# Identity matmuls beside the routing's vector steps, and the first cast of x moved ahead of a register reading

## What is computed

```python
# attention: B, H, S, D = 4, 8, 576, 64; its output x is [4, 576, 512]
logits = np.einsum('bsd,de->bse', x, w_gate)              # 8 experts
local_gate = 1.0 / (1.0 + np.exp(-np.einsum('bsd,de->bse', x, w_local).squeeze(-1)))
for b in range(B):
    prev_e = -1
    for s in range(S):
        fresh_e = int(np.argmax(logits[b, s]))
        if s == 0 or local_gate[b, s] < 0.5:
            e = fresh_e
        else:
            e = prev_e if prev_e >= 0 else fresh_e
        prev_e = e
        # p = softmax(logits[b, s])
        h = np.maximum(x[b, s] @ w1[e], 0.0)              # 512 -> 1024
        out[b, s] = p[e] * (h @ w2[e])                    # 1024 -> 512
```

## Time and profile before

| what | value |
|---|---|
| median of three runs | 727.08 us |
| profiled execution | 727.54 us |
| its span, first to last instruction | 725.7 us |
| mean granted TensorE clock | 0.967 of full speed |
| TensorE matmul / VectorE / ScalarE / GpSimd busy | 91% / 52% / 47% / 27% of the span |

### The profile page before, as it was taken

One profiled execution on the slowest core, in us unless ns is written; L12 is line 12 of the kernel. 1 busy time (PEld: TensorE's weight loads), 2 busy tenths in 40 slices (PEclk: granted clock), 3 DMA queues, 4 the chain that ended last, 5 costly groups with the idle time before them and its releaser, 6 DMA issues. The chain is left out here.

```text
span 725.7 us, 13847 instructions
## 1 busy us (share of the span) xinstructions
PE 657.4 (91%) x4323; PEld 525.1 (72%) x4323; DVE 377.1 (52%) x781; ACT 341.0 (47%) x705; POOL 196.4 (27%) x172
## 2 busy tenths in 40 slices
PE   4776799999999999999955799999999999999994
PEld 1222678888888888888735688888888888888883
DVE  4998465555555555555757632269523432222220
ACT  4896656666666666666530342267424422222221
POOL 3000344444444444445511011113211121111101
PEclk9998999999999999999985699999999999999998
DMA  3997814447544444444074824146411111111100
GB/s 81 209 226 168 180 33 99 99 99 203 111 98 99 99 99 98 98 99 98 16 252 159 304 86 146 43 159 252 146 43 43 36 44 43 43 43 43 43 0 1
DMA packets 68183, 77.04 MB, mean 106 GB/s; under 512 B 46767, under 2 KB 47279, under 8 KB 68144
## 3 DMA queue, kind: packets, MB, share of 16 engines
q1 hardware_dynamic: 63392, 64.58, 34.2%
q0 software_dynamic: 4080, 11.54, 4.9%
q10 hardware_dynamic: 672, 0.44, 0.2%
HBM read 69.06 MB, written 11.27 MB: 111 GB/s over the span
## 5 line engine op out<-in xcount | busy, mean ns | idle before, releaser
L791 DVE CUSTOM_DVE_ANT_0 sm<-ps_s,bias 128x576 f32<-128x576 f32 x128 | 91.7, 754 | 68.8 <-PE ps_s L1063 68.8
L611 ACT ACTIVATE sm<-sm,negmax 128x576 f32<-128x576 f32 x144 | 111.9, 778 | 7.0 <-DVE negmax L791 6.9
L1238 PE MATMUL ps_pv<-w2hi,hThi 128*128 128x512 f32 x200 | 80.5, 402 | 1.3 <-DVEq L980 1.3
L1000 DVE TENSOR_TENSOR hTlo<-ps_s,hThi 128x512 fp32r<-128x512 f32 x50 | 32.2, 686 | 95.1 <-ACT hThi L725 95.1
L1238 PE MATMUL ps_pv<-w2hi,hTlo 128*128 128x512 f32 x200 | 78.3, 392 | 0.0
L1238 PE MATMUL ps_pv<-w2lo,hThi 128*128 128x512 f32 x200 | 78.0, 390 | 0.0
L1134 PE MATMUL ps_pv<-pT,vt 128*64 128x320 f32 (+1 forms) x512 | 69.2, 410 | 4.3 <-DVE pT L814 0.6
L506 POOL CAST ksplit<-raw 128x1152 fp32r<-128x1152 f32 x15 | 17.2, 1146 | 204.8 <-DMA raw<-in_kq_dram 204.8
L1216 PE MATMUL ps_s<-w1hi,xThi 128*128 128x512 f32 x200 | 66.1, 412 | 7.2 <-DVE w1lo L967 3.7
L558 POOL DMA_INDIRECT out_dram<-ysb,sidx x25 | 26.7, 1070 | 153.0 <-ACT ysb L732 153.0
L717 ACT ACTIVATE hsb<-ps_s 128x512 f32<-128x512 f32 x25 | 14.9, 598 | 113.1 <-PE ps_s L1216 113.1
(11 more groups left out here) (180 smaller groups left out, 1279.0 us busy)
## 6 DMA issues: line engine op xcount, KB each, us to landing
w1raw<-in_moe_w_dram SPq DMA_DIRECT2D x18, 1024.0 KB
w2raw<-in_moe_w_dram SPq DMA_DIRECT2D x18, 1024.0 KB
raw<-in_kq_dram SPq DMA_DIRECT2D x32, 432.0 KB, 5.3
bias<-stage SPq DMA_DIRECT2D x32, 288.0 KB, 4.6
raw<-in_kq_dram SPq DMA_DIRECT2D x32, 128.0 KB, 5.1
vt<-in_v_dram SPq DMA_DIRECT2D x32, 128.0 KB, 2.5
tokens_dram<-xl SPq DMA_DIRECT2D x64, 64.0 KB, 1.7
bias_tail<-stage SPq DMA_DIRECT2D x4, 144.0 KB, 2.4
```

Source lines behind the costliest of these rows:

```text
L611: nc.scalar.activation(probs, probs, ACT.Exp, scale=-1.0, bias=negmax[:, u % 2, hd:hd + 1], accum_out=sums[:, pr % 2, 2 * t + hd:2 * t + h ...
L791: nc.vector.tensor_tensor_reduce(sm[:, u % 2, S * hd:S * (hd + 1)].rearrange("p (a c) -> p a c", a=2), ps_s[:, hd, :, 0:HALF], bias.rearra ...
L1000: V.tensor_tensor(hTlo[:, 4 * i:4 * i + 4, :].rearrange("p k t -> p (k t)"), ps_s[:, 1, i, :], hThi[:, 4 * i:4 * i + 4, :].bitcast(F32).re ...
L1238: last = nc.tensor.matmul(ps_pv[:], h[:, f, :], w[:, f, :], start=f == 0 and h is hThi and w is w2hi, stop=f == KF - 1 and h is hTlo)
```

## The change

TensorE gets a helper `beside(first, last, n)`: for each step count from `first` to `last - 1` it waits until `route` has it and then multiplies `ident` by itself, 128x128 in f32, into `ps_pv`, which nothing reads there; at the last count it does so `n` times. It is called ahead of the turn of `hold` (one matmul), ahead of the turn of `code` (three), behind that turn (three and five), and behind the counts (twelve and three). After the 20 probability matmuls of L1193 and ahead of `turn_x(0, 0, 0)` stand twelve more, without waits. The scan that makes `prefix` gets the name `counts`. On ScalarE `xt_hi(0)` and on VectorE `xt_lo(0)` move ahead of the wait for `tiles_told` and the register reading.

```diff
@@ scalar
             split_hi(-1, None, w2_in_e, w2hi, w2raw, w2_hi, None)
+            xt_hi(0)
             act.wait_ge(tiles_told, 1)
...
             split_changed(changed, 0, run, w1_in, w1hi, w1raw, w1_hi, h_done)
-            xt_hi(0)
@@ vector
-                                      0.0, ALU.mult, ALU.add))
+                                      0.0, ALU.mult, ALU.add), "counts")
...
+            xt_lo(0)
             dve.wait_ge(tiles_told, 1)
...
             split_changed(changed, 0, slot, w1hi, w1lo, w1raw, w1_lo, w1_hi, h_done)
-            xt_lo(0)
@@ tensor
+            def beside(first, last, n=1):
+
+                for count in range(first, last):
+                    pe.wait_ge(route, count)
+                    for _ in range(n if count == last - 1 else 1):
+                        nc.tensor.matmul(ps_pv[:, 0:P], ident[:], ident[:], start=True, stop=True)
             pe.wait_ge(tables, 12)
             for n, name, dst, turned in ((1, "hold", ps_t, hold_turned), (0, "code", ps_s[:, 0], codes_turned)):
+                beside(1 if n else AT["hold"] + 2, AT[name])
                 pe.wait_ge(route, AT[name])
...
+            beside(AT["code"] + 3, AT["chosen"], 5)
             pe.wait_ge(route, AT["chosen"])
...
                              start=True, stop=True).then_inc(counted, 1)
+            beside(AT["counts"], AT["places0"], 3)
             for c in range(BT):
...
             last.then_inc(probs_placed, 1)
+
+            for _ in range(12):
+                nc.tensor.matmul(ps_pv[:, 0:P], ident[:], ident[:], start=True, stop=True)
```

## The result

The changed kernel takes **730.21 us**, the median of 17 runs (727.25 to 732.45), against 727.08 for the kernel before on the same occasions (17 runs, 724.95 to 728.94). The ratio is 1.004, with a 95% interval of 1.0025 to 1.0056: slower by 0.4%, where 0.5% (730.7 us) was forecast. The profiled execution took 731.4 us around a span of 729.6; before it was 727.54 around 725.7.

What follows compares the result with a forecast made beforehand. TensorE's first hidden matmul was taken to set the end: 398.96 + 4.3 (twelve fills) - 0.5 (turn) - 0.2 (casts) = 402.6, +3.6 us on 727.08, so 730.7 us; 8-in-10 range 723.6 to 732.0.

Steps and rivals of the forecast that it cites:

- The bound: Expert stage: TensorE's first hidden matmul, at 398.96, sets the end; whatever moves it moves the end as much.
- The price of a fill: Each 128x128 f32 filling matmul on TensorE: 0.22 us at the high clock, 0.43 us at the low.
- Part 1: Fills around the turns of hold and code: the clock falls, slow fills delay the turn of chosen, onehot 1.1 us later.
- Part 2: Fifteen fills behind the counts: no charge, gidx's 0.56 us wait on TensorE disappears; gidx +0.5 us in sum, at 390.3.
- Part 3: Twelve fills ahead of the turn of x: probability matmuls stay at the low clock, the turn starts 4.3 us later.
- Part 4: The turn of x itself: at the high clock behind the fills, 0.6 us in place of 1.11, -0.5 us.
- Part 5: Casts ahead of register readings: VectorE's reading stays in the way, 3.3 us from turn's end against 3.48, -0.2 us.
- Part 6: Clock in tiles 0 and 1: lost in the idle gaps, they pay 2.9 and 2.8 us again; change 0.
- Rival A: Routing: the clock never falls, probability matmuls at half the price; -3.1 us together, 724.0 us; chance 0.29.
- Rival B: Fills' delay paid, but the clock outlives the idle 3.3 us and tile 0 takes 5.5 us; 727.8 us; chance 0.16.

Runs made afterwards that it cites:

- a1: The changed kernel without the twelve fills ahead of the turn of x; 726.87 us, ratio 1.000 to the kernel before.
- a4: The kernel before with only the `beside` fills around the first turns and behind the counts, casts unmoved; 728.33 us, ratio 1.0013.
- c1: The changed kernel with all its fills, but both casts of x moved back behind the register readings; 726.94 us, ratio 1.0007 to the kernel before.
- a3: The kernel before with only the casts of x moved ahead of the register readings; 726.59 us, ratio 0.9998.
- a2: The kernel before with only the twelve fills ahead of the turn of x; 726.12 us, ratio 0.9994.
- d4: The changed kernel with eight more fills behind the turn of x; 728.70 us, ratio 1.0021 to the kernel before.
- d1: The kernel before with only eight fills behind the turn of tile 0's x and fourteen behind tile 0's transposes; 722.71 us, ratio 0.9944.
- b2: The kernel before with only fourteen fills behind tile 0's transposes, ahead of tile 1; 724.89 us, ratio 0.9983.
- b1: The changed kernel without its twelve fills, with eight behind the turn of x and fourteen behind tile 0's transposes; 722.95 us, ratio 0.9956 to the kernel before.

## Why the prediction was right, point by point

- **The bound** (398.96 moves the end). Right: the start of tile 0 moved by 3.62 us, the span by 3.9. Of the 3.62 us, 0.32 came from attention, which the sum (+3.6) did not have; from the routing's first matmul it is 3.3.
- **The price of a fill**, 0.22 and 0.43 us. Right: eight fills took 2.03 us at the high clock from 375.05 to 377.08 (0.25 each, as they wait for steps between), and the twelve 4.98 us, 0.42 each.
- **Part 1**, the clock lost at 373.9 and onehot 1.1 us late. Wrong for the profiled execution, where the clock held and onehot came 0.3 us earlier behind the logits; the judgement that failed there is "I judge no". Right for the other six traces of kernels with these fills, where the clock had fallen by 374.1 (a1 and a4: onehot 1.0 and 1.2 us later). The profiled execution is the exception.
- **Part 2**, gidx at 390.3. It came at 389.38: the 0.56 us of waiting is gone, as said, and Part 1's delay did not come. In c1, where it came, gidx was 0.4 us later behind the logits than in the kernel before (said: 0.5).
- **Part 3**, the decisive one: probability matmuls at the low price in spite of the fills before them (0.214 us each), and the turn at 398.7. It came at 398.67, and the exact agreement is luck: two errors of 0.7 us cancel. The fills began 0.7 us earlier and took 5.0 us instead of 4.3, for the clock came back about 4.7 us into them (398.4) and not after 3.5. The 3.5 was a reading of the row from 70 to 73; the dense work there begins at 69.38 in the trace, so the clock came back after 4.1 us.
- **Part 4**, 0.6 us for the turn. Right.
- **Part 5**, 3.3 us from the turn's end, VectorE's reading in the way. Right (the row's 3.31 us of idle time), and a3 shows the worth of the move as 0.17 us (said: 0.2).
- **Part 6**, tile 0 and tile 1 as before. Right in size (8.56, 8.35) for the profiled execution. But the prediction booked this as no change, where a2, c1 and d4 show that much of the loss lies here: the twelve fills would have given the clock to tile 0 if the moved cast had not made the idle stretch behind the turn long enough to lose it. Of the loss of 0.4% (2.9 us), c1 takes away 2.4 us and d4 1.4. The sum had +4.3 for the fills and -0.2 for the cast; behind the late turn the moved cast is no gain but costs 1.7 us of start (3.91 us from the turn's start against 2.23 in c1) and the clock. Neither part alone shows a cost (0.9994 and 0.9998).
- **Rival A** needed the clock high through the probability matmuls. It was high from 385 and fell at 388.1, in the placing matmuls ahead of them. **Rival B** did not happen in the profiled execution. It happened in a2 and c1, and the five short runs of the changed kernel (727.25 to 727.76 us, clock 0.985) are at its time (727.8), so it probably happened in these too; without a trace that is not shown. The median of 730.21 is then that of a mixture in which the forecast's course had the larger share, and its closeness to 730.7 is in part luck.

## What to carry to other kernels

A fill ahead of awaited work is free only where the engine would wait longer than the fills take at the clock that they will have. Eight fit into 3.48 us even at the low clock (d1: 3.47 us); fourteen fit into 3.71 us only because the clock was high in them (3.29 us in b2; at 0.43 us each it would be 6.0). Put them behind the last work that someone waits for, not ahead of it. Filling has to reach to the start of the dense work that is to profit: an idle stretch between the fills and that work can take back what they bought. And when a step is moved ahead of another on one engine, look for what the other one releases: here a semaphore behind a register reading.

## What the runs showed of the hardware

- Executions of one program differ by several us, and the mean granted clock goes with it. Of the changed kernel's 17 runs the five shortest (727.25 to 727.76 us) have 0.985, the two longest (732.45 and 732.33 us) 0.970 and 0.972. The kernels whose two gaps are filled spread over 0.6 (d1), 1.2 (d2) and 2.1 us (b1), in six runs each.
- A few full-size matmuls between steps did keep the clock at 1.00 for eight us in one execution (373 to 381, TensorE's rows busy for 6.13 of 8.00 us), and in none of the six other traces with the same or nearly the same fills. Why was not tried.
- The 20 matmuls of 52 columns (the probabilities), one behind the other, ran at 0.50 in every trace, from 391.2 on at the latest, also where the clock had been at 1.00 for the whole of the 20 of 26 columns before them (a1, a4, c1).
